# Top-k attention with a gated product on Trainium2: where the low part of the keys is computed

## What is computed

```python
def _attn_ref(q, k, v):                      # (4, 8, 576, 64) each
    scores = scale * np.matmul(q, k.transpose(0, 1, 3, 2))
    kth = np.partition(scores, -top_k, axis=-1)[..., -top_k:-top_k + 1]    # top_k = 32
    mask = scores >= kth
    scores = np.where(mask, scores, -1000000000.0)
    scores = scores - np.max(scores, axis=-1, keepdims=True)
    attn = np.exp(scores)
    attn = attn / (np.sum(attn, axis=-1, keepdims=True) + 1e-09)
    return np.matmul(attn, v)

def _moe_ref(x, w_a, w_b, w_out):            # x: 2304 tokens x 512; 512 x 1536, 512 x 1536, 1536 x 512
    a = x @ w_a
    b = x @ w_b
    return a * b @ w_out
```

## Time and profile before

| | |
|---|---|
| median of 3 runs | 818.16 us (817.97 to 818.72) |
| profiled execution | 817.8 us, of which the profile's span 815.4 us |
| TensorE busy | 771.7 us (95% of the span) |
| VectorE busy | 744.3 us (91%) |
| ScalarE busy | 657.0 us (81%) |
| GpSimd busy | 507.4 us (62%) |
| TensorE's share of the chain that ended last | 86% |

### The profile page before, as it was taken

How to read it: one execution, slowest core, us unless ns; L and a number is a source line. 1 busy time by engine, 2 the same in 40 slices (tenths; PEclk the granted TensorE clock), 3 DMA queues, 4 the chain that set the end, 5 groups by cost and what they waited for, 6 DMA issues and landing times.

```text
span 815.4 us, 18431 instructions
## 1 busy us (share of the span) xinstructions
PE 771.7 (95%) x5952; PEld 686.3 (84%) x5952; DVE 744.3 (91%) x1603; ACT 657.0 (81%) x1614; POOL 507.4 (62%) x560
## 2 busy tenths in 40 slices
PE   5368899999999999999999999999999999999998
PEld 4246788899998989898889899989998889898887
DVE  6999999998999999999999999999999999999500
ACT  5678978888888888888888888888888888888732
POOL 2989986656555666666756565665656555665532
PEclk9957999999999999999999999999999999999999
DMA  6566754445553444444644443544463434343562
GB/s 169 150 186 199 217 185 148 138 137 150 149 167 113 140 125 129 126 138 142 178 142 134 128 137 122 145 136 136 137 183 123 137 124 137 124 133 117 167 214 84
DMA packets 117245, 119.16 MB, mean 146 GB/s; under 512 B 61856, under 2 KB 80288, under 8 KB 117152
## 3 DMA queue, kind: packets, MB, share of 16 engines
q1 hardware_dynamic: 116880, 117.93, 47.8%
q10 hardware_dynamic: 272, 0.07, 0.0%
HBM read 108.53 MB, written 9.44 MB: 145 GB/s over the span
## 4 chain that ended last, share of the span: by engine, by line
PE 86%; POOL 5%; DVE 4%; DMA 2%; issue 2%; ACT 1%; SPq 0%; POOLq 0%; ACTq 0%
PE ps L588 37%; PE ps L620 18%; PE ps L557 10%; PE ps L523 9%; PE ps L539 8%; PE ps L599 3%; DVE best L976 2%; DVE work L993 2%; POOL scores L901 2%; POOL w_lo L856 1%; POOL k_t L856 1%; DMA x_scratch<-k_t 1%; PE ps L492 1%; PE ps L501 1%; DMA stage<-in_w 0%
## 5 line engine op out<-in xcount | busy, mean ns | idle before, releaser
L976 DVE MAX8 best<-work 128x8 f32<-128x576 f32 x432 | 304.4, 747 | 0.0
L901 POOL TENSOR_TENSOR scores<-scores,keep 128x576 f32<-128x576 f32 x144 | 207.0, 1441 | 37.4 <-ACT keep L715 36.6
L993 DVE MATCH_REPLACE8 work<-best,work 128x576 f32<-128x576 f32 x288 | 212.0, 745 | 0.0
L588 PE MATMUL ps<-w_hi,x_hi 128*128 128x384 f32 x576 | 202.5, 351 | 2.4 <-issue 1.2
L588 PE MATMUL ps<-w_hi,x_lo 128*128 128x384 f32 x576 | 194.4, 338 | 0.0
L908 POOL TENSOR_TENSOR ab<-ab 128x384 f32<-128x384 f32 x72 | 73.3, 1018 | 158.6 <-ACT ab L773 158.6
L588 PE MATMUL ps<-w_lo,x_hi 128*128 128x384 f32 x432 | 145.8, 337 | 0.0
L747 ACT COPY probs_t<-ps 128x512 f32<-128x512 f32 x144 | 82.2, 586 | 51.8 <-PE ps L539 49.7
L588 PEld LDWEIGHTS ps<-w_hi,x_hi 128*128 128x128 f32 x576 | 108.1, 188 | 17.5 <-issue 13.9
L724 ACT ACTIVATE scores<-scores,neg 128x576 f32<-128x576 f32 x144 | 114.4, 822 | 6.6 <-POOL scores L901 6.4
L739 ACT ACTIVATE scores<-scores,inverse 128x576 f32<-128x576 f32 x144 | 115.4, 803 | 0.3 <-DVE inverse L1003 0.3
(11 more groups left out here) (64 smaller groups left out, 1300.9 us busy)
## 6 DMA issues: line engine op xcount, KB each, us to landing
wo_lo<-x_scratch SPq DMA_DIRECT2D x69, 768.0 KB, 4.5
wb_lo<-x_scratch SPq DMA_DIRECT2D x70, 384.0 KB, 4.1
stage<-in_w SPq DMA_DIRECT2D x36, 256.0 KB, 3.1
x_scratch<-k_t SPq DMA_DIRECT2D x18, 256.0 KB, 2.4
k_rows<-in_k SPq DMA_DIRECT2D x32, 128.0 KB, 4.7
v_rows<-in_v SPq DMA_DIRECT2D x32, 128.0 KB, 2.6
out<-stage SPq DMA_DIRECT2D x16, 256.0 KB, 4.2
q_rows<-in_q SPq DMA_DIRECT2D x63, 64.0 KB, 3.5
```

Source lines behind the costliest of these rows:

```text
L588: last = mm(ps_ab[which], x[:, g % 2, kb, :], w, start=(kb == 0 and m == 0), stop=(kb == KB - 1 and m == 2))
L901: V.tensor_tensor(row, row, keep[:, j, :], ALU.add).then_inc(mask_done, 1)
L976: ins = V.max(best[:, u % 2, j, 8 * r:8 * r + 8], src)
L993: V.match_replace(out=work[:, j, :], in_to_replace=best[:, u % 2, j, 8 * r:8 * r + 8], in_values=src, imm_value=NEG).then_inc(chain, 1)
```

## The change

From pair 3 on ScalarE makes only the high part. VectorE subtracts it from the keys in PSUM, in two instructions, behind the reciprocal in its step `PREP_SLOT[n] + 1`, and gives the new semaphore `klo_late`. GpSimd's subtraction of these pairs goes. TensorE's `qk` waits for `klo_late`, up to the same pairs for which it waited for the whole copy; for the pairs 1 and 2 all stays.

```diff
--- before.py
+++ after.py
@@ -269,6 +269,7 @@
         k_copied = sem("k_copied")
         klo_first = sem("klo_first")
         klo_ready = sem("klo_ready")
+        klo_late = sem("klo_late")
         qt_done = sem("qt_done")
         qhi_ready = sem("qhi_ready")
         q_copied = sem("q_copied")
@@ -508,8 +509,9 @@
                 pe.wait_ge(qt_ready, u + 1)
                 pe.wait_ge(q_copied, min(u + 2, NU))
                 pe.wait_ge(klo_first, 1)
-                wait(pe, klo_ready, pairs_until(u) - 1)
-                wait(pe, k_copied, sum(m <= u - 2 for m in PREP_SLOT[1:]))
+                wait(pe, klo_ready, min(pairs_until(u), KB - 1) - 1)
+                wait(pe, k_copied, sum(m <= u - 2 for m in PREP_SLOT[1:KB - 1]))
+                wait(pe, klo_late, sum(m <= u - 2 for m in PREP_SLOT[KB - 1:]))
                 wait(pe, s_ready, 2 * u)
                 wait(pe, pt_ready, copied(u - 3))
                 for half in range(2):
@@ -676,7 +678,7 @@
                         act.wait_ge(st_w[m], 16 * len(range(m, len(LEAVING), LOWS)))
                 for frm, a, z in keys_in_psum(n):
                     A.copy(k_t[:, n % KPAIRS, 0, a:z], frm[:, 0:z - a]).then_inc(khi_ready, 1)
-                if n > 0:
+                if 0 < n < KB - 1:
                     wait(act, klo_ready, n - 1)
                     for frm, a, z in keys_in_psum(n):
                         last = A.copy(k_whole[:, a:z], frm[:, 0:z - a])
@@ -860,7 +862,7 @@
                     split_lo(i)
 
             def split_k(n):
-                pool.wait_ge(khi_ready, n + 1 if n < 3 else 3 + 2 * (n - 2))
+                pool.wait_ge(khi_ready, n + 1)
                 pool.wait_ge(k_copied, n)
                 place = n % KPAIRS
                 V.tensor_tensor(k_t[:, place, 1, :], k_whole[:], k_t[:, place, 0, :], ALU.subtract).then_inc(klo_ready, 1)
@@ -928,9 +930,6 @@
                 negate(s - 1)
                 masked(s - 1, 0)
                 masked(s - 1, 1)
-                for m in preps_at(s - 1):
-                    if m >= KB - 1:
-                        split_k(m)
                 if s < NU + 2 or n >= NCH:
                     hidden_lo(n - 2)
                 for m in range(2, 5):
@@ -1008,6 +1007,12 @@
                 V.tensor_scalar(keep[:, j, :], scores[:, u % ROWS, j, 0:S], best[:, u % 2, j, TOPK - 1:TOPK], NEG,
                                 ALU.is_lt, ALU.mult).then_inc(keep_ready[j], 1)
 
+            def split_k(n):
+                dve.wait_ge(khi_ready, 3 + 2 * (n - 2))
+                for frm, a, z in keys_in_psum(n):
+                    last = V.tensor_tensor(k_t[:, n % KPAIRS, 1, a:z], frm[:, 0:z - a], k_t[:, n % KPAIRS, 0, a:z], ALU.subtract)
+                last.then_inc(klo_late, 1)
+
             found, taken = [0, 0], [0, 0]
             for s in range(NU):
                 if s > 0:
@@ -1019,6 +1024,9 @@
                 take_out(s, 1, 0)
                 take_out(s, 1, 1)
                 invert(s - 1)
+                for m in preps_at(s - 1):
+                    if m >= KB - 1:
+                        split_k(m)
                 find(s, 2)
                 take_out(s, 2, 0)
                 take_out(s, 2, 1)
```

## The result

The changed kernel takes 824.26 us (median of 4 runs, 823.86 to 825.95) against 818.07 us for the kernel before (4 runs, 817.77 to 818.72): a ratio of 1.0079, 95% interval 1.0061 to 1.0096. It is slower by 6.2 us. Forecast were 825.3 us and a range of 820.5 to 830.0. The profiled execution took 823.86 us with a span of 822.1, so 6.7 us more span than before.

What follows compares the result with a forecast made beforehand. The prediction took TensorE's queue to bound the kernel from 108 us on. Its terms, 0.8 + 1.9 + 4.4 = 7.1 us, put on the median of 818.16, gave 825.3 us, range 820.5 to 830.0.

Steps and rivals of the forecast that it cites:

- The bound: From 108 us TensorE's queue alone sets the end; whatever it waits for there is added in full.
- what is waited for now: TensorE's score products wait for klo_late, given only behind VectorE's reciprocal in the same step; nearly all the subtraction is exposed.
- step 1: Before 108 us: VectorE's queue, leading the chain, grows by 0.76 us, costing 0.8 us; TensorE's 8.5 us wait is absorbed.
- stop of step 11: Products at 134.84 us, reciprocal at 135.81 with VectorE never idle: TensorE stands for 1.9 us.
- eleven stops: The other steps with a subtraction, such as 13, 31 and 53: TensorE stands 0.40 us in each, 4.4 us.
- The semaphore: Between the subtraction's last result and TensorE's score products: about 0.05 us.
- The relief of ScalarE: Without its whole copy, ScalarE's exponentials and sums_eps come 0.58 us earlier, and so may VectorE's reciprocal.
- Whatever ScalarE or GpSimd save there is worth nothing: From 108 us, time saved on these two engines gains nothing by itself, since TensorE computes 655.05 of 656.00 us.
- Hidden: Rival: the eleven steps cost nothing, 820.5 us, or 818 to 819.5 if all is absorbed; chance 0.07 for nearly whole.
- Faster: Rival: before 108 us GpSimd loses a 1.42 us subtraction in step 1, TensorE starts earlier, 816.8 us; chance 0.03.
- Shared ports: Rival: each of twelve VectorE subtractions waits for a GpSimd instruction of 1.0 us, 837 us; chance 0.06 with other large additions.
- VectorE as the bound: Rival: VectorE gains 9.9 us of work, loses up to 14.2 us of idling from 108 to 764 us; given nothing.

Runs made afterwards that it cites:

- e1: The changed kernel with VectorE's two subtractions in front of the reciprocal instead of behind it; 817.99 us.
- e2: The changed kernel with VectorE's subtractions in front of the two MATCH_REPLACE8 before the reciprocal, some 1.5 us earlier still; 815.52 us.
- e5: The changed kernel with ScalarE's whole copy of the keys put back, though nobody reads it; 831.66 us.
- e4: The kernel before, with GpSimd's subtraction of the keys behind the low part of the hidden layer instead of in front of it; 816.77 us.
- e9: The changed kernel with GpSimd's subtraction alone put back in its old place, into a buffer nobody reads; 825.41 us.
- e8: The changed kernel with pair 3 alone back on ScalarE's copy and GpSimd's subtraction; 824.97 us.
- e3: The changed kernel with ScalarE's whole copy back and VectorE subtracting from it, so TensorE waits for the copy and not for VectorE; 818.49 us.

## Why the prediction was right

**The bound** and **what is waited for now** were right: TensorE stands twelve times in its unbroken stretch, for `klo_late`, and no other wait of it grows. e1 and e2 show it by moving the subtraction and nothing else. The terms of the sum, against the profile:

| term | predicted | profile |
|---|---|---|
| step 1 | 0.8 | 0.1 |
| stop of step 11 | 1.9 | 2.55 |
| eleven stops | 11 x 0.40 = 4.4 | 11 x 0.67 = 7.4 |
| given back in steps 11, 13, 29, 33, 49 | none | -2.7 |
| the wait at 772.5 us of the profile before | none | -0.6 |
| sum | 7.1 | 6.8 |

The sum was right to 0.4 us because errors of nearly 4 us stood against each other. The mechanism was right; that the sum came so close was luck. (The 6.8 us are the difference of two profiled executions; that of the medians is 6.2, against 7.1 forecast.)

**The semaphore.** I put 0.05 us between the subtraction's end and the products. It was 0.36 in step 31 (350.25 to 350.61) and in step 11 (137.11 to 137.47). The 0.31 us too few cover the error of the eleven stops (0.27 us each) and half of that of step 11 (0.65); the other half is VectorE's lateness of 0.4 us, which the prediction had put into the term of step 1. A row that warned of it stood in the trace of before: in step 1 the copy that released TensorE ended at 18.56 and the products started at 18.81, so 0.25 us from ScalarE.

**The subtractions.** Forecast 0.43 and 0.49 us, measured 0.41 and 0.49 (13 each). The relief of ScalarE, 0.58 us forecast, was 0.53 in step 31 and 0.6 in e5. One sign did not come as forecast: VectorE's waits for `sums_eps`, which were to fall well below 14.2 us, only fell to 12.2. The relief is in them, but TensorE's stops give VectorE new idle time; with ScalarE's copies back, in e5, they are 18.9. First the changed kernel (108 to 770 us), then e5 (108 to 775).

```profile
DVE inverse L1002 <- ACT sums_eps L734: 12.2, 15, 1.5
```

```profile
DVE inverse L1002 <- ACT sums_eps L734: 18.9, 15, 1.9
```

**"Whatever ScalarE or GpSimd save there is worth nothing"** was wrong. It rested on 655.05 busy us of 656, and busy rows hold waits of some tenths: e4 only moves GpSimd's subtraction behind the low part, and TensorE regains 2.7 us. The step of the working that failed here is that GpSimd's subtraction was waited for by nobody: ScalarE's copy waited for it, through the hidden layer's low part. It did no harm to the sign, since the loss was the larger.

**Step 1.** TensorE was only 0.1 us late at step 10, but that is one execution: e5 and e9, with the same work of VectorE in step 1, had 0.6 and 0.9. VectorE was 0.4 us late at step 11. That lateness of TensorE at the start is no cost of its own, because in step 11 it waits for VectorE anyway, was right, and e1 agrees; VectorE's lateness is passed on. Step 1 and the stop of step 11 together were forecast as 2.7 us and came to 2.65; in e8, without VectorE's work in step 1, to 2.4, and in e9 to 3.15.

**The rivals.** Hidden: no, for the eleven stops. Faster: in the changed kernel no, but the 2.7 us that e4 wins from step 11 on are a gain of that kind, at another place than I had it. Shared ports: no, and e3 shows what it would have been. VectorE as the bound: no; in e2 it does the same work in a kernel that is faster than before.

## What to carry to other kernels

Handing an operation to an engine moves the semaphore too: ask where in the new engine's queue it stands, and when its buffer is wanted again. Here 1.5 us earlier in the same queue turned a loss of 6.2 us into a gain of 2.3, with the same work. A wait of 10.8 us where the bound engine had time cost nothing that could be measured, and eleven of 0.6 us where it had none cost 7.

## What the runs showed of the hardware

In the profile of the changed kernel the end of VectorE's second subtraction and the start of the score products that it releases lie 0.36 us apart in ten of the twelve stops from step 11 on, 0.41 in the other two and 0.25 in step 1.

VectorE's subtraction with both inputs in SBUF took 2.94 us for a pair beside GpSimd, 0.42 and 0.48 us when GpSimd was idle, and from PSUM 0.84 us for the pair beside GpSimd (e3 and the changed kernel, step 1).

TensorE's granted clock was 0.67 to 0.73 over a stretch of 4 us, soon after TensorE had stood for 1.9 to 2.5 us, in four profiles (e1, e3 and e4 from 110 us, e8 from 138), and it stayed at 1.00 in others with such a stop (the changed kernel at 137 us, e2 at 108). What decides it these runs don't show.
